# Gated linear attention, token and channel mixing on one core: channel loop over pairs of hidden tiles, score products and last channel terms on 64-row tiles of TensorE, five PSUM banks for single products

## The reference

```python
for t in range(S):                       # per batch and head
    m_new = max(f[t] + m, i[t])
    C = exp(f[t] + m - m_new) * C + exp(i[t] - m_new) * outer(v[t], k[t])
    n = exp(f[t] + m - m_new) * n + exp(i[t] - m_new) * k[t]
    y[t] = sigmoid(o[t]) * (C @ q[t]) / max(abs(n @ q[t]), 1.0)
# x: y as (B, 768, 320)
h  = relu(x.T @ w_tok1) @ w_tok2         # token mixing, hidden size 256
u  = x + h.T
x2 = u + relu(u @ w_ch1) @ w_ch2         # channel mixing, hidden size 1536
gate = sigmoid(causal 5-tap convolution of x2 over the tokens)
out = (gate * (x2 @ w_val)) @ w_out
```

## Time and profile before

| what | value |
|---|---|
| median of 3 runs | 309.8 us (307.46 to 310.57) |
| span of the profiled execution, first to last instruction | 308.2 us |
| median minus span | 1.6 us |
| TensorE (PE) busy | 270.8 us, 88% |
| VectorE (DVE) busy | 210.7 us, 68% |
| ScalarE (ACT) busy | 121.9 us, 40% |
| GpSimd (POOL) busy | 89.4 us, 29% |
| mean granted clock | 0.966 |

### The profile page before, as it was taken

One profiled execution on the slowest core, in us unless ns is written; L12 is line 12 of the kernel. 1 busy time (PEld: TensorE's weight loads), 2 busy tenths in 40 slices (PEclk: granted clock), 3 DMA queues, 4 the chain that ended last, 5 costly groups with the idle time before them and its releaser, 6 DMA issues.

```text
span 308.2 us, 5374 instructions
## 1 busy us (share of the span) xinstructions
PE 270.8 (88%) x2024; PEld 258.5 (84%) x2024; DVE 210.7 (68%) x415; ACT 121.9 (40%) x224; POOL 89.4 (29%) x102
## 2 busy tenths in 40 slices
PE   0876765884999999999999999999999999999854
PEld 0765654783998999999899999999999999999754
DVE  7999999977778687576677740352774138763693
ACT  4344453432874453434434223323123333231623
POOL 4537445554046445334610400000004000040340
PEclk9999598796899999999999999999999999999999
DMA  7599833344547554242000001000000010000011
GB/s 223 158 309 310 241 128 83 100 170 144 169 128 217 141 155 117 66 136 65 2 0 0 3 0 66 0 0 2 0 2 1 32 34 0 2 0 1 23 43 64
DMA packets 26289, 25.70 MB, mean 83 GB/s; under 512 B 13976, under 2 KB 22008, under 8 KB 26264
## 3 DMA queue, kind: packets, MB, share of 16 engines
q1 hardware_dynamic: 21976, 18.72, 20.9%
q10 hardware_dynamic: 4288, 6.64, 6.5%
HBM read 23.34 MB, written 2.02 MB: 82 GB/s over the span
## 4 chain that ended last, share of the span: by engine, by line
PE 60%; DVE 17%; issue 7%; ACT 6%; DMA 4%; POOL 3%; SPq 1%; ACTq 0%; DVEq 0%; POOLq 0%
PE shared L1171 25%; PE h_ps L1309 18%; DVE prob L933 7%; PE s_ps L1209 3%; DVE gate L1037 2%; PE hv_ps L1190 2%; PE shared L1274 2%; PE s_ps L1246 2%; PE hv_ps L1194 2%; PE shared L1230 2%; DVE y_lo L942 1%; DMA G_all<-G_scratch 1%; PE shared L1259 1%; DMA stage<-val 1%; DMA stage<-wout 1%
## 5 line engine op out<-in xcount | busy, mean ns | idle before, releaser
L933 DVE SCALAR_TENSOR_TENSOR prob<-G_all,A_col,mask_sb 128x128 f32<-128x128 f32 x96 | 51.3, 602 | 0.2 <-DMA G_all<-G_scratch 0.2
L1101 DVE SCALAR_TENSOR_TENSOR h_lo<-shared,h_hi 128x384 fp32r<-128x384 f32 x48 | 26.5, 557 | 35.0 <-ACT h_hi L826 34.8
L1309 PE MATMUL h_ps<-ch_hi,h_hi 128*128 128x320 f32 x144 | 45.4, 315 | 0.0
L1309 PE MATMUL h_ps<-ch_hi,h_lo 128*128 128x320 f32 x144 | 44.5, 309 | 0.0
L826 ACT ACTIVATE h_hi<-shared 128x384 fp32r<-128x384 f32 x48 | 23.1, 488 | 53.8 <-PE shared L1171 50.8
L1309 PE MATMUL h_ps<-ch_lo,h_hi 128*128 128x320 f32 x144 | 44.3, 308 | 0.0
L697 ACT ACTIVATE prob<-prob 128x512 f32<-128x512 f32 x24 | 15.0, 631 | 48.5 <-DVE prob L933 48.4
L1171 PE MATMUL shared<-u_hi,ch_hi 128*128 128x384 f32 x96 | 32.9, 342 | 0.6 <-DVE yt L982 0.4
L1171 PE MATMUL shared<-u_lo,ch_hi 128*128 128x384 f32 x96 | 32.5, 339 | 0.0
L1171 PE MATMUL shared<-u_hi,ch_lo 128*128 128x384 f32 x96 | 32.5, 338 | 0.0
L1037 DVE SCALAR_TENSOR_TENSOR gate<-x,conv_sb,gate 128x384 f32<-128x384 f32 x44 | 29.0, 668 | 1.0
(11 more groups left out here) (189 smaller groups left out, 620.6 us busy)
## 6 DMA issues: line engine op xcount, KB each, us to landing
G_all<-G_scratch SPq DMA_DIRECT2D x11, 512.0 KB, 4.8
o_sig<-on ACTq DMA_DIRECT2D x2, 960.0 KB, 6.1
k_in<-kT SPq DMA_DIRECT2D x24, 80.0 KB
q_in<-qT SPq DMA_DIRECT2D x24, 80.0 KB
kn_in<-kn SPq DMA_DIRECT2D x12, 160.0 KB, 3.9
v_in<-vn SPq DMA_DIRECT2D x12, 160.0 KB, 4.6
stage<-ch ACTq DMA_DIRECT2D x3, 640.0 KB, 4.4
out<-o_sb SPq DMA_DIRECT2D x12, 160.0 KB, 1.8
```

The costliest lines, as they stand in the source:

```text
L933: last = dve.scalar_tensor_tensor(out=prob[(2 * u + g) % 4][:, tile_cols(j)], in0=G_all[u % 2][:, tile_cols(h)], scalar=A_col[:, col:col + ...
L1101: took(dve.scalar_tensor_tensor(out=h_lo[i % 3][:], in0=ps_of(key)[:, 0:T], scalar=0.0, in1=h_hi[i % 3][:].bitcast(F32), op0=ALU.max, op1= ...
L1309: last = pe.matmul(h2_ps[t][:, 0:DM], a[:, tile_cols(t)], w[:, f, :], start=(f == 0 and n == 0), stop=(f == FT - 1 and n == 2))
```

## The change

The channel loop goes over six pairs of hidden tiles (`PAIRS`), in seven steps. A step issues both tiles of a pair; then the attention, turns, value or output products of the step; then `channel_out` for the two tiles of the pair before. In the pair, each tile has its first seven matmuls; the eighth, with `u_lo` and the stacked weights, runs on 64 rows only: rows 0 to 63 for the even tile, rows 64 to 127 for the odd one, into two banks, one right behind the other. Only the high part of the weights is used in it, so the stacked weights of the odd tiles have their high part in rows 64 to 127 and their rest in rows 0 to 63. The score products run on rows 0 to 39 and 64 to 103 in turn, the two groups alternating, and `k_in` has one plane and needs no zeros. The state's increment alternates the groups as well. `x2` of blocks 0 and 2, value products, and the output products of blocks 0 and 1 take the banks of `s_ps` and `hv_ps`, which are free by then; the others take the two shared banks in turn. Four `h_hi`/`h_lo` buffers replace three.

```diff
-LAG = 2
-STEPS = FT + LAG - 1
-ATT_AT = {0: 0, 2: 1, 4: 2, 6: 3, 8: 4, 10: 5, 11: 6}
-TURN_AT = {2: (0, 1), 3: (2,)}
-VAL_AT = {8: 0, 9: 1, 10: 2}
+PAIRS = FT // 2
+STEPS = PAIRS + 1
+TURN_AT = {1: (0, 1, 2)}
+VAL_AT = {4: (0,), 5: (1, 2)}
...
+def banks_of(jobs):
+    bank, use, count, turns = {}, {}, [0] * 5, 0
+    for key in jobs:
+        name, n = key[0], key[1]
+        if key == ("y", NU - 1):
+            b = 2
+        elif name == "x2" and n in (0, 2) or name == "val" and n < NQ - 1 or name == "out" and n < NQ - 2:
+            b = 2 + key[2]
+        elif name in ("val", "out") and n == NQ - 1:
+            continue
+        else:
+            b, turns = turns % 2, turns + 1
...
-                    for g in range(2):
-                        w = 2 * u + g
-                        if w >= 2:
-                            pe.wait_ge(prob_ready, w - 1)
-                        for j in range(HG):
-                            last = pe.matmul(s_ps[g][:, tile_cols(j)], k_in[k_buffer(u)][:, g, tile_cols(j)],
-                                             q_in[k][:, tile_cols(j)], start=True, stop=True)
-                        last.then_inc(s_ready, 1)
+                    if u >= 1:
+                        pe.wait_ge(prob_ready, 2 * u)
+                    for j in range(HG):
+                        for g in range(2):
+                            r = slice(64 * g, 64 * g + D)
+                            last = pe.matmul(s_ps[g][:, tile_cols(j)], k_in[k_buffer(u)][r, tile_cols(j)],
+                                             q_in[k][r, tile_cols(j)], start=True, stop=True)
+                    last.then_inc(s_ready, 2)
...
+            def channel_hidden(q, fs):
+                x_hi, x_lo = u_hi[q % 2], u_lo[q % 2]
+                for f in fs:
+                    ps = begin(("ch1", q, f))
+                    terms = over_model(ch1_hi, ch1_lo, ch1_st, tile_cols(f), x_hi, x_lo)[:-1]
+                    for n, (w, x) in enumerate(terms):
+                        pe.matmul(ps[:, 0:T], w, x, start=(n == 0), stop=False)
+                for f in fs:
+                    r = slice(64 * (f % 2), 64 * (f % 2) + 64)
+                    pe.matmul(ps_of(("ch1", q, f))[:, 0:T], ch1_st[r, tile_cols(f)], x_lo[r, 2, :],
+                              start=False, stop=True).then_inc(shared_full, 1)
...
+                for p in range(STEPS):
+                    if p < PAIRS:
+                        channel_hidden(q, (2 * p, 2 * p + 1))
+                    if q == 0:
+                        attention(1, p)
...
+                    if 1 <= p < PAIRS:
+                        channel_out(q, (2 * p - 2,))
+                        channel_out(q, (2 * p - 1,))
+                    elif p == PAIRS:
+                        channel_out(q, (FT - 2, FT - 1))
```

More of the change, by code:

```diff
@@ L273, in build @@
         shared_full = sem("shared_full")
-        shared_done = [sem(f"shared_done{k}") for k in range(2)]
+        bank_done = [sem(f"bank_done{k}") for k in range(5)]
         hi_ready = sem("hi_ready")
@@ L635, in _ @@
             make_lo(pool, 5, 1)
-            for i in range(STEPS):
-                if i in ATT_AT:
-                    attention(1, ATT_AT[i])
+            for p in range(STEPS):
+                attention(1, p)
             for q in range(NQ):
@@ L1366, in _ @@
                     if q > 0:
+                        for e in range(ET):
+                            done(pe, ("out", q - 2, e))
                         for c in range(NC):
@@ L1418, in _ @@
             project(q - 1, 2)
+            for d in range(3):
+                done(pe, ("val", q - 1, d))
             pe.wait_ge(x2_lo_ready, TT * NQ)
```

194 lines of the change are left out of this document (94 added, 100 removed).

## The result

The changed kernel takes 318.66 us (median of 4 executions, 318.15 to 319.83). The kernel before, beside it, takes 308.75. The ratio is 1.030, with a 95% interval of 1.024 to 1.037. The change makes the kernel slower, by about 10 us; 2.9 of these were forecast, and the time lies outside the range. The profiled execution has a span of 318.0 us against 308.2, so 9.8 us are to be found.

The account below looks back on a forecast made before the run. DVE was taken to bound batch 0's attention, PE everything from the first channel loop to 287 us. Block 0 to the mark -1.9, sixteen pairs +2.4 and stalls +2.4 made +2.9: 312.8 us, range 305.5 to 317.

Parts of the forecast that it names:

- Scores: Attention score products: two row groups in turn run side by side, 0.87 us less per unit.
- Rival B: Score products: weight loads run serially, so scores gain nothing; 315.5 us in all, chance 0.22.
- Last terms: Half-row last products of each hidden-tile pair: changing tile shape costs more than the saved matmul, +0.15 us per pair.
- Rival C: Hidden-tile pairs: changing to row tiles is free, -0.17 us per pair; 306.0 us in all, chance 0.25.
- Stalls at the second pair: Second pair of blocks 2 and 3: PE waits for the first pair's h_lo, 1.2 us net each, +2.4 together.
- Banks and steps of convolutions by pairs: Five banks, and convolutions coming whole into a step: no gain or loss in blocks 2 and 3, zero.
- Block 0: First channel loop with batch 1's attention: unit 7's increment at 98.2, then three cycles of 9.66 us, to 127.2.
- The mark in block 1: End of the first two channel_out in block 1: 157.0 against 159.00 before, -1.9 us.
- the weights' chain: End of block 0: val and wout loads, last division and block 1's first h_lo all move by -1.1 us.
- From block 1's second tile to the mark: Block 1 from tile 2 at 150.5: a pair 2.8, three turns 1.0, two channel_out 2.7, ending at 157.0.
- Ahead of the loop: Batch 0's attention, 20 to 66 us: DVE bounds, so no gain; a change over 0.5 us would show it wrong.
- four cases: Main forecast 312.8 us (0.40); serial loads 315.5 (0.22); free shape changes 306.0 (0.25); free changes with serial loads 309.9 (0.08).

Follow-up runs that it names:

- POOL's wait: Changed kernel, but in the second batch POOL weighs a unit's values only after DVE has made that unit's exponents: 314.05 us, ratio 1.007.
- Tile by tile, POOL's wait: Changed kernel with each tile's eight products together on all 128 rows, and POOL waiting for DVE's exponents in the second batch: 307.99 us, ratio 0.991.
- mask in PSUM: Exponents' mask in PSUM for units 0 to 6: changed kernel 311.48 us; kernel before 304.50; changed kernel with whole tiles together and POOL waiting for DVE 303.84.

## Why the prediction was wrong

**Scores: right.** 0.87 us per unit was forecast, 0.89 measured. Rival B (loads one after another) falls. The cycle of block 0 was forecast at 9.66 us and is 9.51 where nothing disturbs it (108.80 - 99.29), 9.53 with POOL's wait.

**Last terms: right, a little small.** +0.15 per pair stood in the sum, 0.21 was measured, inside the bound of 0.25. Rival C (free changes) falls. Where they lie:

```profile
219.94 0.34 PE L1316 MATMUL shared<-u_hi,ch_st 128*128 128x384 f32 x1
220.21 0.44 PE L1319 MATMUL shared<-u_lo,ch_st 64*128 64x384 f32 x2
220.58 0.41 PE L1336 MATMUL h_ps<-ch_hi,h_hi 128*128 128x320 f32 x1
220.82 0.31 PE L1336 MATMUL h_ps<-ch_lo,h_hi 128*128 128x320 f32 x1
```

From the last full product to the second of `channel_out` are 220.82 - 219.94 = 0.88 us. With whole products they would be three steps of 0.173 and one of 0.147, 0.67. The first half product comes 0.27 behind the last full one instead of 0.17, as in the earlier trace rows. The two half products and the change out take 0.37, where two whole ones take 0.35, so nothing is left of what their overlap brings. And the first full product pays 0.24 instead of 0.15, as in the earlier trace rows.

**Stalls at the second pair: right.** 1.2 net each was forecast, 1.28 measured.

```profile
215.94 0.44 PE L1319 MATMUL shared<-u_lo,ch_st 64*128 64x384 f32 x2
217.55 0.44 PE L1316 MATMUL shared<-u_hi,ch_hi 128*128 128x384 f32 x1 [1.17 <-DVE h_lo L1117]
...
216.42 0.87 ACT L843 ACTIVATE h_hi<-shared 128x384 fp32r<-128x384 f32 x2 [2.56 <-PE shared L1319]
...
216.94 1.02 DVE L1117 SCALAR_TENSOR_TENSOR h_lo<-shared,h_hi 128x384 fp32r<-128x384 f32 x2 [2.50 <-ACT h_hi L843]
```

Banks and steps of convolutions by pairs are worth 95.23 - 95.53 = -0.3 us over blocks 2 and 3; zero stood in the sum.

**Block 0: wrong, and this is the step that failed.** "DVE keeps up: it is idle 1.96 in its round" took DVE's durations as fixed. They depend on where POOL stands. The third increment behind unit 7's was forecast at 127.2. It came at 131.90, with a wait of 2.41 us at the one before it and, behind that wait, 1.6 us lost at the lower clock. The mark in block 1 moved with it, to 163.23 against 157.0 forecast and 159.00 in the earlier trace rows, and so did the weights' chain, here in its order after:

```profile
138.86 3.80 DMA stage<-val
...
146.31 3.25 DMA stage<-wout
...
153.45 0.04 DVE yt L999
```

With POOL's wait and all else of the change the forecast points are met: unit 7's increment comes at 98.34 (98.2 forecast), the third behind it at 126.90 (127.2), DVE's `h_lo` behind the last division at 149.41 (150 forecast), and PE waits for it 2.36 us and starts tile 2 at 149.93 (150.5). So the plan of that step was right up to there, but for the stop that it didn't know.

**From block 1's second tile to the mark: wrong as well, by 1.7 us.** From tile 2 to the mark 6.5 us were forecast (157.0 - 150.5). It took 163.23 - 154.99 = 8.24 in the changed kernel and 158.14 - 149.93 = 8.21 with POOL's wait. Both have the granted clock at 0.50 for three microseconds there, behind PE's wait for `h_lo` (from 156 and from 151 us). "Tile by tile, POOL's wait" has a wait as long (2.40) and no such stretch, and takes 156.15 - 149.62 = 6.53. The forecast priced PE's wait and took the products behind it at full clock; why the clock falls behind one such wait and not behind the other isn't shown.

The stretch from the loop's start to the end of block 1 is 102.09 - 103.02 = -0.9 us against the kernel before with POOL's wait. I had forecast -1.3. That these are so near is partly luck: the 1.7 us at the lower clock are in the one and not in the other, and the rest came out 1.3 better than forecast.

**Ahead of the loop: wrong by its own test, and the test was too sharp.** I wrote that a change of more than 0.5 us there would prove me wrong. It was +1.56 in the profile that was compared. Five profiles with the old score products and the mask in SBUF start the loop at 84.29 to 87.89, and eleven with the new ones at 84.52 to 88.08, so the offset can't be told from scatter. Without the stops of the exponents the three profiles with the mask in PSUM start at 79.48 to 81.51; whether the stops make the scatter too isn't shown.

**The sum.** Forecast +2.9: -1.3 and +4.2. In the profile +9.8: +1.56 before the loop (not told from scatter), -0.9 for the middle stretch by itself, +4.4 for the shut-out (some 2.5 of it PE's longer cycle, 1.6 the lower clock behind it), +4.8 for pairs and stalls. None of the four cases had an exclusion of two engines in it, or a fall of the clock in block 0. Yet the profile before showed it, in the exponents' group from 20 to 66 us (busy us, mean ns): 878 ns on the mean, where the median of the line is 343 and the longest takes 3537.

```profile
L933 DVE SCALAR_TENSOR_TENSOR prob<-G_all,A_col,mask_sb 128x128 f32<-128x128 f32 x34 | 27.6, 878 | 0.0
```

## What to carry to other kernels

Where instructions of one form show a median of 0.34 us and single ones of 3.5, lay the other engines' timelines beside the long ones before counting on that engine's idle time. In this kernel a VectorE operation with both inputs in SBUF stood for whole GpSimd instructions. Give it one input from PSUM, or order the two engines by a wait. A faster step moves loads against the other engines' work: ask what these release, and beside what it will then run. And a wait of PE can cost more than its length: look at the granted clock of the stretch behind it.

## What the runs showed of the hardware that I had not expected

Of the 96 instructions of the exponents (two inputs of 128x128 in SBUF), 25 took longer than 0.45 us in the changed kernel and 22 in the kernel before. Each of these 47 ended 0.14 to 0.16 us after an instruction of POOL. Mostly a DVE instruction stands for one of POOL's. Seven stood for three, 3.28 to 3.56 us: four in the changed kernel, three in the kernel before, each time over `kept`, `qs` and the lower part behind them. Why they got no turn between those I can't say. POOL loses little: `kept` takes 0.51 us beside a standing DVE instruction, 0.47 otherwise.

With the mask in PSUM eight exponents start 0.27 us apart, with POOL's `y` and weighing beside them from 41.25 us on:

```profile
41.09 2.15 DVE L935 SCALAR_TENSOR_TENSOR prob<-G_all,A_col,h_ps 128x128 f32<-128x128 f32 x8
43.15 3.73 DVE L999 COPY apart<-state 64x164 f32<-64x164 f32 x2
```

A DVE copy from SBUF to SBUF was shut out as well (3.73 us for two that take 0.48), though it has one input. The Trainium skill (SBUF — State Buffer, Who interferes with whom) lists `copy` among the operations that can take both ports. The trace agrees.

In the kernel before the granted clock is 1.00 from the first channel loop to 300 us. In the changed kernel it is 0.50 for about three microseconds twice (from 122 and from 156 us), each time behind a wait of PE of 2.4 us. A product of 320 columns then starts 0.27 us behind the one ahead instead of 0.15, which costs 1.6 to 1.7 us each time, on top of the wait.

Products on 40 rows in two row groups cost 0.068 us apiece in turn (1.09 / 16), 0.102 group by group, 0.124 on 128 rows with the changes of shape at both ends included.
